# Moving two attention units by one half step, reordering the prologue, and adding 1e-9 inside a reduction

## The reference

```python
scores = scale * np.matmul(q, k.transpose(0, 1, 3, 2))      # 4 x 8 x 576 x 576, head size 64
scores = np.where(masks[None, :, :, :], scores, -1000000000.0)
scores = scores - np.max(scores, axis=-1, keepdims=True)
attn = np.exp(scores)
attn = attn / (np.sum(attn, axis=-1, keepdims=True) + 1e-09)
attn_out = np.matmul(attn, v)

h = x @ w_in                                                 # x: 2304 x 512, w_in: 512 x 2048
g = np.where(h >= 1, h, np.where(h <= -1, 0.0, (h + 1) ** 2 / 4))
y = g @ w_out                                                # w_out: 2048 x 512

do_compute = (y @ w_skip) > 0                                # rows with a positive score
# those rows: out = y + gate * (relu(y @ w1[e]) @ w2[e]) of their expert e, the others: out = y
```

## Time and profile before

| | |
|---|---|
| median of 3 runs | 508.34 us (508.17 to 508.83) |
| profiled execution | 509.94 us, its span 508.1 us (1.84 us lie around the span) |
| PE busy | 497.4 us, 98% of the span, 3423 matmuls |
| PE weight loads (overlap PE) | 428.7 us, 84% |
| DVE / ACT / POOL busy | 260.7 / 195.5 / 213.2 us |
| L1411, clip, 96 times | mean 554 ns |
| L1668, square, 96 times | mean 617 ns |
| chain that ended last | PE 85%, DVE 9%, issue 2%, ACT 2% |

### The profile page before, as it was taken

The page is one execution under the profiler, slowest core; times in us unless marked ns, Lnnn a source line. Parts: engine busy times, 40 slices in busy tenths (PEclk is TensorE's granted clock), DMA queues, the critical chain, the costliest instruction groups (busy, mean ns, idle before and its releaser), DMA issues.

```text
span 508.1 us, 8892 instructions
## 1 busy us (share of the span) xinstructions
PE 497.4 (98%) x3423; PEld 428.7 (84%) x3423; DVE 260.7 (51%) x594; ACT 195.5 (38%) x435; POOL 213.2 (42%) x235
## 2 busy tenths in 40 slices
PE   8899999899999999999999999999999999999996
PEld 5577888789998888888888888888998899888895
DVE  5967557744335525676643676762435242332322
ACT  4776564462223334434332434433322222322222
POOL 0669777662223235455523546551222322222221
PEclk9799999999999999999999999999999999999999
DMA  8993202101101204020310420000210008750001
GB/s 254 337 386 136 76 2 79 53 2 72 54 0 50 73 23 168 13 73 32 97 48 0 173 80 18 17 1 19 88 37 1 1 9 323 275 182 1 2 1 65
DMA packets 18977, 42.15 MB, mean 83 GB/s; under 512 B 2054, under 2 KB 3920, under 8 KB 18932
## 3 DMA queue, kind: packets, MB, share of 16 engines
q1 hardware_dynamic: 18836, 41.54, 23.8%
q0 software_dynamic: 96, 0.02, 0.0%
HBM read 32.94 MB, written 8.78 MB: 82 GB/s over the span
## 4 chain that ended last, share of the span: by engine, by line
PE 85%; DVE 9%; issue 2%; ACT 2%; POOL 0%; DVEq 0%; ACTq 0%
PE bank L1029 36%; PE bank L1045 36%; PE bank L868 4%; PE bank L831 3%; PE bank L848 3%; DVE row_sum L1190 1%; PE bank L812 1%; DVE row_max L1168 1%; DVE x_lo L1200 1%; ACT x_hi L1575 1%; DVE row_sum L1193 1%; PE bank L972 1%; PE bank L953 1%; DVE act_f L1411 1%; DVE bank L1173 1%
## 5 line engine op out<-in xcount | busy, mean ns | idle before, releaser
L1780 POOL TENSOR_TENSOR g_lo<-act_f,g_hi 128x384 fp32r<-128x384 f32 x96 | 97.4, 1014 | 196.9 <-ACT g_hi L1677 196.5
L1668 ACT ACTIVATE act_f<-act_f,half_col 128x384 f32<-128x384 f32 x96 | 59.3, 617 | 201.5 <-DVE act_f L1411 201.5
L1411 DVE TENSOR_SCALAR act_f<-bank 128x384 f32<-128x384 f32 x96 | 53.2, 554 | 143.2 <-PE bank L1029 135.0
L1029 PE MATMUL bank<-x_hi,win_hi 128*128 128x384 f32 x384 | 87.8, 348 | 0.6 <-DVE act_f L1414 0.6
L1045 PE MATMUL bank<-wout_hi,g_hi 128*128 128x512 f32 x285 | 85.1, 407 | 0.0
L1677 ACT CAST g_hi<-act_f 128x384 fp32r<-128x384 f32 x96 | 49.4, 514 | 91.5 <-DVE act_f L1414 91.3
L1029 PE MATMUL bank<-x_hi,win_lo 128*128 128x384 f32 x384 | 83.9, 337 | 0.0
L1029 PE MATMUL bank<-x_lo,win_hi 128*128 128x384 f32 x384 | 83.1, 334 | 0.0
L1045 PE MATMUL bank<-wout_lo,g_hi 128*128 128x512 f32 x285 | 81.0, 392 | 0.0
L1045 PE MATMUL bank<-wout_hi,g_lo 128*128 128x512 f32 x285 | 81.0, 392 | 0.0
L1029 PEld LDWEIGHTS bank<-x_hi,win_hi 128*128 128x128 f32 x384 | 66.6, 188 | 8.5 <-issue 1.5
(11 more groups left out here) (129 smaller groups left out, 431.1 us busy)
## 6 DMA issues: line engine op xcount, KB each, us to landing
w_early<-in_w_dram SPq DMA_DIRECT2D x4, 2048.0 KB, 8.8
qk<-in_qk_dram SPq DMA_DIRECT2D x12, 592.0 KB, 4.6
out_dram<-y_rows SPq DMA_DIRECT2D x18, 256.0 KB, 2.6
win_raw<-in_w_in_dram SPq DMA_DIRECT2D x16, 256.0 KB, 9.3
wout_raw<-in_w_out_dram SPq DMA_DIRECT2D x16, 256.0 KB, 9.8
y_dram<-y_rows SPq DMA_DIRECT2D x15, 256.0 KB, 3.0
v<-in_v_dram SPq DMA_DIRECT2D x6, 384.0 KB
v<-in_v_dram SPq DMA_DIRECT2D x6, 288.0 KB
```

The costliest lines, as they stand in the source:

```text
L1029: mm = pe.matmul(h_ps[s % 2][:, 0:CH], w[:, f, P * k:P * (k + 1)], x[:, k, cols], start=(at == 0), stop=(at == len(order) - 1))
L1411: dve.tensor_scalar(tile, h_ps[s % 2][:, 0:CH], -1.0, 1.0, ALU.max, ALU.min).then_inc(clip_ready, 1)
L1668: act.activation(tile, tile, ACT.Square, bias=half_col[:, 0:1], scale=0.5).then_inc(square_ready, 1)
L1780: pool.tensor_tensor(g_lo[:, s % RING, :], act_f[:, s % 2, :], g_hi[:, s % RING, :].bitcast(F32), ALU.subtract).then_inc(g_lo_ready, 1)
```

## The change

Four things are changed.

1. The strings of the prologue. On PE, P1 comes ahead of S5, P2 ahead of V0, and V3 ahead of P4; four fillers are added ahead of P1. On DVE, E2 comes ahead of M4, and E5 ahead of the first L. On ACT, unit 5's exponentials come after C3. Its banks move with the order on PE.
2. Unit 5's maxima are subtracted by GpSimd (job D5, L1718 of the changed kernel) behind G3; ACT then takes unit 5's exponentials with two ACTIVATEs of 72x288 in place of eight of 72x72.
3. Everywhere, the row sums of a unit go to `sum_terms`, an array with pairs of places whose second one was filled with 1e-9 once at the start; the TENSOR_SCALAR that added 1e-9 becomes a TENSOR_REDUCE that adds each pair.
4. In the first chunk, units 8 and 12 are placed at half steps 7 and 20 instead of 6 and 21. For unit 8 all five jobs move one half step later; for unit 12, S, X and E one half step earlier, while P and V stay.

```diff
+SHIFTED = 5
...
-PE_BEFORE = "S0 S1 S2 S3 S4 P0 S5 P1 V0 P2 V1 P3 V2 P4 V3 P5 V4 V5"
-DVE_BEFORE = "M0 M1 E0 M2 E1 M3 M4 E2 E3 M5 E4 L0 E5 L1 L2 L3 L4 L5"
-ACT_BEFORE = "X0 X1 X2 C0 X3 C1 X4 C2 H0 X5 C3 H1 W0 H2 C4 H3 C5 H4 H5 W1 W2"
-POOL_BEFORE = "G0 G1 G2 G3 G4 G5 R0 R1 R2"
...
+PE_BEFORE = "S0 S1 S2 S3 S4 P0 P1 S5 P2 V0 V1 P3 V2 V3 P4 P5 V4 V5"
+DVE_BEFORE = "M0 M1 E0 M2 E1 M3 E2 M4 E3 M5 E4 E5 L0 L1 L2 L3 L4 L5"
+ACT_BEFORE = "X0 X1 X2 C0 X3 C1 X4 C2 H0 C3 X5 H1 H2 W0 H3 C4 C5 H4 H5 W1 W2"
+POOL_BEFORE = "G0 G1 G2 G3 D5 G4 G5 R0 R1 R2"
...
+FILLERS = {("P", 0): 4, ("S", 1): 4, ("S", 2): 9, ("P", 1): 4, ("P", 2): 5, ("P", 3): 2, ("P", 4): 2, ("P", 5): 2, ("V", 4): 2}
...
-        for i, at in enumerate((6, 10, 14, 17, 21, 24)):
-            unit_at(N_PRO + REST + i, at, 5, 7)
+        for i, at in enumerate((7, 10, 14, 17, 20, 24)):
+            unit_at(N_PRO + REST + i, at, 6 if i == 4 else 5, 8 if i == 4 else 7)
...
+        sum_terms = sb("sum_terms", [TQ, 2, 4, 2], F32)
...
-                    dve.tensor_reduce(sums_of(u, hh), tiled(u, hh), AX.X, ALU.add).then_inc(sum_steps, 1)
+                    dve.tensor_reduce(sum_terms[0:unit_rows(u), hh, 0:u.nt, 0], tiled(u, hh), AX.X, ALU.add)\
+                       .then_inc(sum_steps, 1)
...
-                dve.tensor_scalar(sums, sums, 1e-9, None, ALU.add).then_inc(sum_steps, 1)
+                dve.tensor_reduce(sums, sum_terms[0:unit_rows(u), :, 0:u.nt, :], AX.X, ALU.add).then_inc(sum_steps, 1)
...
+            dve.memset(sum_terms[:, :, :, :], 1e-9).then_inc(terms_ready, 1)
+            dve.wait_ge(terms_ready, 1)
...
-                    if n < N_PRO:
+                    if SHIFTED <= n < N_PRO:
+                        act.wait_ge(first_shift_ready, 2 * (n - SHIFTED) + hh + 1)
+                        a = act.activation(prob_of(u, hh), prob_of(u, hh), ACT.Exp)
+                    elif n < SHIFTED:
...
-                        .then_inc(shift_ready, 1)
+                        .then_inc(first_shift_ready if n < N_PRO else shift_ready, 1)
...
+                if kind == "D":
+                    shift_scores(n)
```

More of the change, by code:

```diff
@@ L104, in pair_last @@
     return u.t0 + u.nt == (8 if strided(u.p) else 6)
-PE_BEFORE = "S0 S1 S2 S3 S4 P0 S5 P1 V0 P2 V1 P3 V2 P4 V3 P5 V4 V5"
-DVE_BEFORE = "M0 M1 E0 M2 E1 M3 M4 E2 E3 M5 E4 L0 E5 L1 L2 L3 L4 L5"
-ACT_BEFORE = "X0 X1 X2 C0 X3 C1 X4 C2 H0 X5 C3 H1 W0 H2 C4 H3 C5 H4 H5 W1 W2"
-POOL_BEFORE = "G0 G1 G2 G3 G4 G5 R0 R1 R2"
-FILLERS = {("P", 0): 4, ("S", 1): 4, ("S", 2): 9, ("P", 2): 5, ("P", 3): 2, ("P", 4): 2, ("P", 5): 2, ("V", 4): 2}
+PE_BEFORE = "S0 S1 S2 S3 S4 P0 P1 S5 P2 V0 V1 P3 V2 V3 P4 P5 V4 V5"
[3 more added lines that the diff above has]
+FILLERS = {("P", 0): 4, ("S", 1): 4, ("S", 2): 9, ("P", 1): 4, ("P", 2): 5, ("P", 3): 2, ("P", 4): 2, ("P", 5): 2, ("V", 4): 2}
 def jobs_of(names):
@@ L437, in build @@
         mask_l_loaded, mask_s_loaded = sem("mask_l_loaded"), sem("mask_s_loaded")
-        half_ready = sem("half_ready")
+        half_ready, terms_ready = sem("half_ready"), sem("terms_ready")
         warm_ready = sem("warm_ready")
@@ L451, in build @@
         masked_ready = sem("masked_ready")
+        first_shift_ready = sem("first_shift_ready")
         shift_ready = sem("shift_ready")
```

## The result

The kernel after took 509.79 us, the median of 21 runs (509.26 to 510.35); beside them the kernel before took 508.57 us (21 runs, 507.92 to 510.06). The ratio is 1.0022, 95% interval 1.0016 to 1.0028: 0.2% slower, where 507.0 us was forecast.

A forecast was written before the change was run, and what follows sets the result against it. PE bounds the kernel from 95 us on; only the prologue and 3.06 us of earlier PE waits can give. -1.2 - 0.4 + 1.4 - 1.0 = -1.2, with a restart saved -1.3: 508.34 - 1.3 = 507.0 us, range 505.4 to 509.6.

The forecast's parts named there:

- the memset costed at nothing: Start of DVE's stream: the one memset lies in idle time before the first scores and was given no cost.
- the prologue's gain of 1.2 us: Ahead of the main loop: hidden(0) begins near 29.7 instead of 30.89 us, -1.2 us.
- run in parallel to the end: After the first chunk, from 95 us on: no difference between the two kernels was expected.
- the same fall: Prologue of the kernel before: TensorE at about half clock between 17 and 24 us, claimed to cost next to nothing there.
- Clock: Prologue: P1 to P3 run at full clock from 17 us on.
- the rival (0.24): Prologue: the clock falls all the same, hidden(0) begins at 32.3, total 509.7 us; chance 0.24.
- Unit 5: Prologue: two ACTIVATEs end its exponentials at 25.2, not 26.36; reciprocal starts at 25.9, not 27.09, 1.2 us earlier.
- the third rival: Prologue bound elsewhere (L3, low weights or H5 late): it gives 0.2 us, total 508.1 us; chance 0.18.
- Unit 8: First chunk: 0.95 us wait ahead of S8 goes, P7 waits 0.35 plus 0.2 restart; balance -0.4 us.
- P9: First chunk: moving V8 behind hidden(7) makes P9's second head wait 1.2 us, with restart +1.4 us.
- unit 12: First chunk: P11's 1.52 us wait goes (1.7 with restart), S12 waits 0.7; balance -1.0 us.
- The 1e-9: Row sums on DVE: 0 on the path; bounds 0.3 us lost and nothing gained beyond the waits counted.

The follow-up runs named there:

- the run with eight more: Kernel after with eight MEMSETs more at the start of DVE's stream: 508.00 us, ratio to before 0.9979.
- sum_alone: Kernel before with only the 1e-9 edit and eight MEMSETs more at the start of DVE's stream: 508.16 us, ratio 0.9984.
- sum_as_before: Kernel after with the 1e-9 added as before by TENSOR_SCALAR and without the MEMSET of sum_terms: 507.91 us, ratio to before 0.9974.
- the prologue alone: Kernel before with only the order strings, the four fillers and D5 put in: 508.72 us, ratio 0.9995.
- v8_back: Kernel after with the 1e-9 as before and V8 kept ahead of hidden(7), where it was before the change: 506.79 us, ratio 0.9954.
- exp_in_eight: Kernel after with the 1e-9 as before, D5 removed and unit 5's exponentials as eight ACTIVATEs: 511.53 us; five of 12 runs at 508.70.
- after_four_more: Kernel after with four MEMSETs more at the start of DVE's stream: 509.85 us.

## Why the prediction was wrong

Two steps failed: the memset costed at nothing, and the prologue's gain of 1.2 us, counted against an execution with the clock fallen.

The one that turned the sign is the last sentence: "After the first chunk the two kernels should run in parallel to the end." PE's work did, to `left_i`. Behind the branch the one memset, costed at nothing because it "lies in DVE's idle time", moved the branch's target into the bad place. The term is +1.9 us (509.79 - 507.91; 1.8 by the run with eight more). I had counted what the added instruction does, not where it puts those behind it. Without that term the kernel after takes 507.9 us, 0.9 us over the forecast and 0.1 over its own range of 506.2 to 507.8, and that nearness is partly luck: as the second step shows, its prologue is not shorter than that of before at the full clock.

The second is the size of the prologue's term, and what it was subtracted from. "Before, the same fall cost next to nothing, because unit 5's eight ACTIVATEs did not wait for PE": wrong. ACT's order puts C2 ahead of them, and in the fall C2 waited for PE (kernel before; in `sum_alone` C2 begins at 21.1 us without a wait):

```profile
23.14 0.88 ACT L1567 COPY prob_t<-bank 72x288 f32<-72x288 f32 x2 [1.48 <-PE bank L848]
```

`hidden(0)` comes at 28.7 us with the full clock and at 30.9 without it, and the run is 1.45 us longer (509.87 - 508.42). The forecast gain of 1.2 us was made against an execution with the clock fallen, and then taken off a median that stands for those without. Against them the new order gains nothing at `hidden(0)` (29.05 or, in `sum_as_before`, 28.5 us against 28.7), and the prologue alone costs 0.3 us (508.72 against 508.42), about the 0.4 us by which its end is longer (below). What it does bring is that no execution has the clock fallen, and four fillers bring that too. That the profiled execution lay 1.6 us above the median was the sign, and the prediction named it without asking why.

The rest, step by step:

- Clock: it stayed at 1.00, as forecast, and the rival (0.24) did not come. The rule that spoke for the rival, that a transpose does not count for the clock gate as a matmul does (the Trainium skill, TensorE: Matmul & The Clock Gate, Part 4), is neither shown nor refuted: four fillers beside the transposes were enough.
- Unit 5: exponentials by 24.6 (forecast 25.2), reciprocal 25.34 (25.9), `hidden(0)` 29.05 (29.7). The relative gain was larger than 1.2, the absolute one none. D5 was in time, and L3 and H5 were too: the third rival did not come, though its effect, a prologue that gives little, did, through another cause.
- Unit 8, P9, unit 12: the waits were forecast within 0.2 us each, their sum at 0. By the waits it is -0.3 us (0.41 + 1.21 + 0.52 - 0.95 - 1.52), by the runs -0.5.
- P9: `v8_back` took 1.1 us off (507.91 - 506.79), the wait of 1.21 less 0.1. The mechanism (V8's `x_lo` ahead of unit 10's masked scores) is shown.
- The 1e-9: nothing in the time of the kernel after (508.00 with it and eight MEMSETs more, 507.91 without), though the end is 0.4 us longer with the MEMSETs, so that a gain of that size is not excluded. In the old places half a microsecond at P11: there "I take 0 on the path" was wrong, since it looked at the readers of the sums and not at the clip that stands behind them on DVE.

The terms by their own runs, from before's 508.42 with the full clock: -0.5 (units), +0.3 (prologue), +1.9 (code behind the branch) give 510.1 us, against 509.79 measured; 0.3 us are within the intervals of the runs that the terms are taken from.

One difference stays open. In the kernels with D5, SP's DRAIN comes 1.5 to 1.6 us behind its branch, in those without it 1.1 (with eight MEMSETs 1.9), since the last rows of the output take that much longer to be stored. An instruction packet lies among them (503.2 us in the kernel after; before had it at 495.3). `exp_in_eight`, without D5, has the packet at 497.0 and SP's DRAIN at 1.1 again. That ACT's stream, six instructions shorter with D5, moves the packet there, and that the packet delays the stores, are guesses that were not tried by themselves.

## What to carry to other kernels

Where a program ends, or goes on, behind a taken branch over much code, read each engine's first instruction behind it: here one instruction more ahead of the target cost 2 us, and eight further ones, or one fewer, gave them back. Before a profiled execution is used as the base of a sum, ask why it differs from the median; here its clock had fallen where half of the runs' had not. Moving a job past a neighbour is decided by who stands behind it on the engine that gives the bank back, and here that could be read from the rows to 0.2 us.

## What had not been expected of the hardware

- An instruction that never runs costs 1.7 us between the medians, 2.7 us by the rows, where it shifts the target of a taken branch (3.8 us instead of 0.5 on DVE). Five instructions more are as bad as one, nine are good. The first instruction packet behind the branch starts about 1 us after it in the good kernels too (0.6 in `after_four_more`, 0.9 to 1.2 in all others); the good ones go on without waiting for it.
- The same order and the same idle time ahead of P1 let TensorE's clock fall in a part of the executions and not in the others: both profiled executions of before had it at half (1.2 GHz) from 17 to 24 us behind 0.84 and 0.85 us of idle time, `sum_alone` kept 2.4 GHz behind 0.84. 14 of 29 runs of before had the mean of 0.993 that goes with the fall. Four matmuls of 128x512 bf16 ahead of P1 kept it at 2.4 GHz in the profile, and the mean at 0.998 or more in all 12 runs.
